# The opening loads of an attention, experts and SoLU kernel: which queue issues the counts and v, and how many warm-up products run before q and k arrive

## What is computed

```
scores = q k^T / sqrt(D) - slope[h] * distance, kept where key < n_global
         or 0 <= query - key < n_local               B=2 H=8 S=768 D=64
attn   = softmax(scores) v
x      = sum_e p[e] * (relu(attn w1[e]) w2[e])       1536 x 512, E=4, F=1024
h      = x w_in;  solu = h * softmax(h);  ln = normalised solu * g_ln
out    = ln w_out                                    1536 x 512
```

## Time and profile before

| | us |
|---|---|
| median of 3 runs | 753.35 (753.34 to 753.66) |
| the profiled execution | 753.5 |
| its span, first to last instruction | 751.7 |
| TensorE busy | 744.6 |
| VectorE busy | 525.5 |
| GpSimd busy | 341.0 |
| ScalarE busy | 218.9 |

### The profile page before, as it was taken

The page is one execution under the profiler, slowest core; times in us unless marked ns, Lnnn a source line. Parts: engine busy times, 40 slices in busy tenths (PEclk is TensorE's granted clock), DMA queues, the critical chain, the costliest instruction groups (busy, mean ns, idle before and its releaser), DMA issues. The chain is left out here.

```text
span 751.7 us, 12616 instructions
## 1 busy us (share of the span) xinstructions
PE 744.6 (99%) x3994; PEld 652.9 (87%) x3994; DVE 525.5 (70%) x1042; ACT 218.9 (29%) x414; POOL 341.0 (45%) x326
## 2 busy tenths in 40 slices
PE   9999999999999999999999999999999999999998
PEld 8888899899898998989988898898898877888876
DVE  5677767676666766767666676676767799867772
ACT  5677641111111111111211112111113743433332
POOL 4367546253542535425354253543535974442400
PEclk9999999999999999999999999999999999999999
DMA  9756310100101000010000100000022100000001
GB/s 263 194 142 167 105 31 2 56 29 29 31 26 56 28 28 28 28 56 28 28 28 28 56 28 28 28 28 0 1 112 66 49 0 15 15 29 28 16 28 42
DMA packets 39106, 37.15 MB, mean 49 GB/s; under 512 B 14497, under 2 KB 31905, under 8 KB 39073
## 3 DMA queue, kind: packets, MB, share of 16 engines
q1 hardware_dynamic: 37472, 34.64, 15.0%
q10 hardware_dynamic: 1600, 2.10, 0.8%
HBM read 33.59 MB, written 3.15 MB: 49 GB/s over the span
## 5 line engine op out<-in xcount | busy, mean ns | idle before, releaser
L809 PE MATMUL y_ps<-w2s,hs 128*128 128x512 f32 x1140 | 286.0, 395 | 0.1
L789 PE MATMUL p_ps<-xs,ws 128*128 128x384 f32 x1344 | 255.2, 336 | 0.0
L809 PEld LDWEIGHTS y_ps<-w2s,hs 128*128 128x128 f32 x1140 | 212.4, 188 | 41.0 <-DVE acc L1474 0.6
L789 PEld LDWEIGHTS p_ps<-xs,ws 128*128 128x128 f32 x1344 | 237.6, 188 | 11.0
L1474 DVE SCALAR_TENSOR_TENSOR acc<-y_ps,pr,acc 128x512 f32<-128x512 f32 x178 | 133.0, 748 | 79.6 <-PE y_ps L809 78.6
L1121 ACT ACTIVATE hs<-hs_sum 128x384 fp32r<-128x384 f32 x128 | 67.4, 527 | 353.6 <-DVE hs_sum L1442 238.9
L1461 DVE SCALAR_TENSOR_TENSOR hs<-hs_sum,hs 128x384 fp32r<-128x384 f32 x128 | 93.2, 737 | 4.3 <-ACT hs L1121 2.2
L577 POOL TENSOR_TENSOR ws_sum<-raw_sum 128x256 f32<-128x256 f32 x16 | 11.8, 739 | 146.8 <-PE p_ps L789 146.0
L608 POOL CAST w2s<-raw_sum 128x1024 fp32r<-128x1024 f32 x16 | 16.9, 1056 | 86.1 <-PE y_ps L809 86.1
L1134 ACT ACTIVATE neg_s<-neg_s,row 128x256 f32<-128x256 f32 (+1 forms) x96 | 42.2, 483 | 26.0 <-DVE row L1493 25.9
L1493 DVE CUSTOM_DVE_ANT_0 neg_s<-s_ps,bias 128x256 f32<-128x256 f32 (+1 forms) x96 | 34.3, 399 | 20.2 <-PE s_ps L823 18.1
(11 more groups left out here) (152 smaller groups left out, 971.2 us busy)
## 6 DMA issues: line engine op xcount, KB each, us to landing
raw_sum<-in_w SPq DMA_DIRECT2D x28, 512.0 KB, 3.5
qk<-in_qkW SPq DMA_DIRECT2D x24, 256.0 KB, 3.7
qk<-in_qkW SPq DMA_DIRECT2D x24, 128.0 KB, 4.1
v_sb<-in_v SPq DMA_DIRECT2D x16, 192.0 KB, 3.0
out<-o_sb SPq DMA_DIRECT2D x12, 256.0 KB, 2.0
raw_sum<-in_w ACTq DMA_DIRECT2D x4, 512.0 KB, 7.0
raw_sum<-in_w_in SPq DMA_DIRECT2D x1, 2048.0 KB, 8.0
wout_lo_a_sum<-in_w_out SPq DMA_DIRECT2D x1, 1792.0 KB, 7.6
```

The lines of the kernel that those rows point to most:

```text
L789: mm = nc.tensor.matmul(bank, ws[slot][:, w, part, kk, :], xs[:, 2 * bt + kk, x, part, :], start=(kk == 0 and w == 1 and x == 1), stop=(kk ...
L809: mm = nc.tensor.matmul(mixed_at(s, t), hs[bt][:, h, b, tok], w2s[slot][:, w, f, :], start=(f == 0 and h == 1 and w == 1), stop=(f == 1 an ...
```

## The change

The counts and the four loads of v of the first round move from SyncE's queue to ScalarE's, where they are issued ahead of everything else, in that order. SyncE's queue now begins with the q/k tiles, all six in a row. The warm-up has 10 products in place of 12.

```diff
-WARM_UP = 12
+WARM_UP = 10
...
         @block.sync
         def _(sp):
-            sp.dma_start(words[:, :], counts_in.bitcast(I32).partition_broadcast(P)).then_inc(words_loaded, 16)
-
             def load_qk(r, b):
...
             for b in range(BL):
                 load_qk(b // STEPS_PAIR, b)
-                if b % STEPS_PAIR == 0:
-                    load_v(b // STEPS_PAIR, b // STEPS_PAIR)
             sp.dma_start(gain_sb[:, :], gain).then_inc(gain_loaded, 16)
             sp.dma_start(pr_raw[:, :, :], probs).then_inc(probs_loaded, 16)
...
         @block.scalar
         def _(act):
+            act.dma_start(words[:, :], counts_in.bitcast(I32).partition_broadcast(P)).then_inc(words_loaded, 16)
+            for p in range(PAIRS):
+                for m in range(2):
+                    act.dma_start(v_sb[:, p, m, W:W + QB, 0:D], v[2 * p + m].rearrange("(i p) d -> p i d", p=P)
+                                  ).then_inc(v_loaded[p], 16)
+
             def load_first_weights(g):
```

## The result

The changed kernel takes 754.81 us (median of 18 runs, 754.67 to 754.97) against 753.41 us for the kernel before on the same chips (18 runs, 753.29 to 753.88): a ratio of 1.0017, with an interval of 1.0011 to 1.0023. It is slower, by 1.4 us, which lies above the forecast range and just under the 1.5 us that I had called the limit of what can be told.

What follows compares the result with a forecast made beforehand. VectorE's chain from the counts was taken to bound the start, TensorE the rest; warm-up, q and k, counts and v at 0 each against 753.5 us, with the median 0.15 us lower, gave 753.4 us, range 752.8 to 754.3 us.

Steps and rivals of the forecast that it cites:

- What bounds the start: First attention step: VectorE, started by the counts' landing, ends TensorE's last wait, not the warm-up or q and k.
- The warm-up, worth 0: Start of TensorE: two products fewer free it 0.57 us sooner, but VectorE's tiles do not move, so 0.
- my four passes in 0.57 us: End of the warm-up: the last four passes read as 0.14 us each, against 0.211 us for the first 18.
- q and k first on their queue, worth 0: SyncE's queue: q/k tiles issued sooner, tile 1's 0.23 us wait replaced by the wait for VectorE, so 0.
- The counts on ScalarE's queue: Start of VectorE's chain: same issue at 0.74 us, landing +0 to +0.8 us, taken as 0.
- The third rival: Counts' landing: late beside q and k or by a later issue, +0.3 to +0.8 us, 753.7 to 754.3 us; 18%.
- ScalarE's issues: ScalarE's queue: four v issues end near 3.3 us, ahead of its first work, so 0.
- my worst case of 6.6 us: ScalarE's four v issues at SyncE's longest issue, 1.36 us each, end at 6.6 us; felt by about 0.3 us.
- The clock, 5%: TensorE near the start: more idle time lowers its rate, costing 1.4 to 2.1 us, 754.9 to 755.6 us; 5%.

Runs made afterwards that it cites:

- warm12: The changed kernel with the warm-up put back from 10 to 12 products; 754.71 us, ratio to before 1.0016.
- warm10: The kernel before with a warm-up of 10 products in place of 12 and nothing else; 753.34 us, ratio 0.9998.
- after_warm17: The changed kernel with 17 warm-up products in place of 10; 754.74 us, ratio 1.0015.
- counts_alone: The kernel before, but SyncE waits for the counts to land before it issues anything else; 754.87 us in one execution.
- counts_act_v_sp: The kernel before with the counts alone moved to ScalarE's queue, v staying on SyncE's; 753.64 us, ratio 1.0002.
- counts_sp_v_act: The changed kernel with the counts back at the head of SyncE's queue, v staying on ScalarE's; 756.02 us, ratio 1.0029.
- v_act_warm17: The changed kernel with the counts back at the head of SyncE's queue and 17 warm-up products in place of 10; 754.53 us, ratio 1.0014.
- both_wait: The changed kernel, but SyncE and ScalarE both wait for the counts to land before they issue anything else; 757.05 us in one execution.
- v_waits: The changed kernel, but ScalarE waits for the counts to land before it issues v; 755.63 us, ratio 1.0035.

## Why the prediction was wrong

**What bounds the start: right.** VectorE's chain from the counts sets the end of step 0. In the eight profiled executions in which the scores came in time, with VectorE starting on the counts at 3.76 to 5.18 us, it is 3.37 to 3.42 us from its first instruction on the counts to its first tile, and the branch is 0.52 to 0.57 us of it. In the others the scores came later than that and set its start.

**The warm-up, worth 0: right.** All three runs that changed it alone in the kernel before or the changed one (`warm12`, `warm10`, `after_warm17`) stayed within 0.15 us of their base by the medians. Its rate was read wrongly, twice. I had the passes speed up near 5.2 us "whatever their number". In the trace of the change the first scores, at 7.04 us, ran at the high rate, but with a warm-up of 10 the scores at 5.55 us ran at the low one in two profiles; and the passes speed up from 4.2 us on in `counts_alone`, while in `counts_act_v_sp` all 24 are slow and the scores at 6.41 us begin so. And a pass at the high rate begins 0.11 us after the one ahead, half of 0.21 us, not 0.14 us: my four passes in 0.57 us counted the whole length of the last.

**q and k first on their queue, worth 0: wrong, hidden by the next.** I bounded tile 0's landing by bytes at the old rate, "by about 6.0 us"; it landed at 6.95 us. The old rate did not hold: by 6.9 us less was moved in total, and v took 0.37 MB of it. v's part is what counts: in `counts_sp_v_act` both queues moved 1.07 MB by then, more than before, 0.55 MB of it v, and q and k came no sooner. Tile 1, forecast for 6.5 to 7.5 us with its wait gone, landed at 9.6 us, and the wait for it was 0.35 us, longer than before; only the late VectorE hid that. By `v_act_warm17` this costs 0.8 us in the trace and 1.1 us by the medians, where the counts are not the bound.

**The counts on ScalarE's queue, taken at 0 with +0 to +0.8 us: this is the step that failed.** It measured +1.3 us (4.4 less 3.1 us), and goes to the end microsecond for microsecond: +1.27 us at VectorE's first tile, +1.3 us in the span. I took 0 "because at 0.74 us the engines are still idle", and bounded the other end by the 3.9 us of a small load that stood in one busy queue, though the change makes two. The 3.9 us bounds nothing: in the changed kernel the same gain load took 7.8 us. The third rival had the right case, the counts late because loads flow beside them, at 18%, with a price of 0.3 to 0.8 us, too cheap by half a microsecond. That they are late by taking turns at the DMA engines, as it says, is not shown: `counts_alone` and `both_wait` show that the company does it, but the engines were less busy than before (18.7% against 24.0% by 3.84 us), and the way stays open. The Trainium skill, "DMA: Bandwidth & Descriptors", section "Queues, rings and completion order", has the DMA engines take turns between queues; the runs agree in direction (3.1 us at the head of one queue, 3.5 us with the other queue loaded beside it), and only they give the size.

**ScalarE's issues: right here, by luck.** Four took 4.79 us, until 6.00 us, inside my worst case of 6.6 us. But I had the table load follow the issues at once, and it follows 0.87 us later, at 6.87 us, as in `v_waits` (8.80 to 9.67 us) and `both_wait` (6.76 to 7.63 us). So the issues, and not `short`, let ScalarE go on, by 0.1 us. It cost nothing only because the counts were late: the table load ended at 8.15 us, ahead of an exponential at 8.89 us but behind the 7.62 us of the kernel before, by an estimated 0.5 us had the counts been in time. `v_waits` shows the same issues 3 us later costing 2 us.

**The clock, 5%:** not what happened in the changed kernel, but real: with hardly more idle time (1.78 us) it cost 1.5 us in `counts_sp_v_act` by the medians, and 2.8 us in its profiled execution. That the prediction's 1.4 us is near the first is luck: it rests on the 0.14 us, and with 0.11 us the same sum gives 2.0 us (4.2 x (1 - 0.11/0.211)).

## What to carry to other kernels

Follow the smallest load that starts the longest chain: here 16 bytes of counts, on whose landing every engine's branch hangs, and each microsecond of which is one of the end. A second queue did not bring it in sooner; it put loads beside it, where the others had all stood behind it in the only queue. When loads are spread over queues, size each landing with both queues full, and ask what stands behind the issues on the engine that now makes them.

## What the runs showed of the hardware

- The same 2 KB broadcast took 2.5 us to land alone, 2.7 us with v behind it, 3.0 to 3.1 us with q, k and v behind it, 3.5 us with q and k beside it, 3.5 us with v beside and q and k behind it, and 4.0 to 4.4 us with q and k beside and v behind it. The loads' effects do not add, and its queue alone makes no difference.
- The passes of the warm-up run at a low rate of 0.21 us each and then at 0.11 us although the granted clock is recorded as 1.00 throughout; 24 of them took 4.29 to 5.20 us in different executions. After 20 passes and 1.7 to 1.8 us of idle time, the next work ran at the high rate in one execution and at the low rate in another. There only the durations of passes show it; in `both_wait`, after 2.69 us of idle time and 0.93 us of scores at the high rate, the granted clock is recorded at 0.50 for about three microseconds.
- Four issues of 192 KB in rows of 256 bytes took ScalarE 3.4 to 4.8 us while q and k were being issued by SyncE, against 1.03 us for two on a single queue, and 2.59 us for four when q and k were issued only near their end.
- From the end of `short`, or of the last issue if that is later, to ScalarE's table load it was 0.85 to 0.87 us in the kernel before, the changed kernel and `v_waits`; on VectorE a branch on the same flag took 0.52 to 0.57 us.
